# Seven block products for eight in the w_in matmuls of a Fourier layer with two feed-forward layers

## The reference

```python
X = np.fft.rfft(x, axis=1); Xr, Xi = X.real, X.imag
Yr = Xr @ w_r - Xi @ w_i + b_r
Yi = Xr @ w_i + Xi @ w_r + b_i
Y  = soft(Yr, 0.01) + 1j * soft(Yi, 0.01)      # sign(v) * max(|v| - 0.01, 0)
x1 = np.fft.irfft(Y, n=3008, axis=1).reshape(6016, 256)

h = x1 @ w_in                                   # 256 x 2048
x2 = (max(h, 0) + alpha * min(h, 0)) @ w_out    # 2048 x 256
h = x2 @ w_in2
out = where(h >= 1, h, where(h <= -1, 0, (h + 1)**2 / 4)) @ w_out2
```

## Time and profile before

| | |
|---|---|
| median of 3 runs | 1272.91 us (1272.61 to 1273.23) |
| profiled execution | 1272.96 us, of which 1271.4 us span |
| TensorE busy | 98% of the span, mean granted clock 0.992 |
| VectorE, ScalarE, GpSimd busy | 62%, 51%, 5% |

### The profile page before, as it was taken

The page is one execution under the profiler, slowest core; times in us unless marked ns, Lnnn a source line. Parts: engine busy times, 40 slices in busy tenths (PEclk is TensorE's granted clock), DMA queues, the critical chain, the costliest instruction groups (busy, mean ns, idle before and its releaser), DMA issues.

```text
span 1271.4 us, 17546 instructions
## 1 busy us (share of the span) xinstructions
PE 1242.4 (98%) x6304; PEld 1095.8 (86%) x6304; DVE 785.7 (62%) x1389; ACT 649.9 (51%) x1312; POOL 68.4 (5%) x86
## 2 busy tenths in 40 slices
PE   6799999999999999999999999999999999999997
PEld 2689988888888888888888888888888888889997
DVE  2477755666665665666656656666566566666675
ACT  2345455555455455554554554545545545555553
POOL 1355500000000000000000000000000000000000
PEclk9799999999999999999999999999999999999999
DMA  8888810000000000000010000000000000000000
GB/s 262 260 257 258 251 41 16 16 1 1 16 3 29 1 16 16 1 16 16 1 31 1 16 16 1 16 17 1 28 1 13 4 1 16 1 1 16 1 16 28
DMA packets 26684, 54.11 MB, mean 43 GB/s; under 512 B 3018, under 2 KB 15562, under 8 KB 26604
## 3 DMA queue, kind: packets, MB, share of 16 engines
q1 hardware_dynamic: 20660, 31.49, 8.6%
q0 software_dynamic: 4576, 15.67, 3.7%
q10 hardware_dynamic: 1372, 5.97, 1.3%
HBM read 34.37 MB, written 18.74 MB: 42 GB/s over the span
## 4 chain that ended last, share of the span: by engine, by line
PE 96%; DMA 2%; DVE 0%; issue 0%; ACT 0%; SPq 0%; ACTq 0%; POOLq 0%
PE bank L890 82%; PE bank L826 5%; PE bank L873 2%; PE bank L801 2%; PE bank L812 2%; PE bank L836 2%; PE bank L884 1%; DMA x_sb<-x 1%; DMA slots_scratch<-a_sb 1%; DMA gc<-group_consts 1%; SPq L386 0%; ACT act_a L601 0%; PE bank L954 0%; DVE g_sb L753 0%; DVE g_sb L756 0%
## 5 line engine op out<-in xcount | busy, mean ns | idle before, releaser
L890 PE MATMUL bank<-x_hi,w_hi 128*128 128x470 f32 (+1 forms) x832 | 314.8, 378 | 0.9 <-DVE x_lo L716 0.9
L890 PE MATMUL bank<-g_hi,w_lo 128*128 128x470 f32 (+1 forms) x832 | 311.2, 374 | 0.0
L890 PE MATMUL bank<-x_hi,w_lo 128*128 128x470 f32 (+1 forms) x832 | 310.6, 373 | 0.0
L890 PE MATMUL bank<-g_lo,w_hi 128*128 128x470 f32 (+1 forms) x832 | 310.2, 373 | 0.0
L890 PE MATMUL bank<-g_hi,w_hi 128*128 128x470 f32 (+1 forms) x832 | 309.4, 372 | 0.8 <-DVE x_lo L770 0.5
L890 PE MATMUL bank<-x_lo,w_hi 128*128 128x470 f32 (+1 forms) x832 | 308.7, 371 | 0.0
L748 DVE SCALAR_TENSOR_TENSOR g_sb<-act_a,neg_alpha,g_sb 128x470 f32<-128x470 f32 (+1 forms) x208 | 145.8, 701 | 229.6 <-ACT g_sb L599 229.3
L727 DVE TENSOR_TENSOR g_lo<-g_sb,g_hi 128x470 fp32r<-128x470 f32 (+1 forms) x416 | 263.5, 633 | 0.1
L601 ACT ACTIVATE act_a<-bank,half 128x470 f32<-128x470 f32 (+1 forms) x208 | 135.0, 649 | 245.7 <-PE bank L890 245.7
L596 ACT ACTIVATE act_a<-bank 128x470 f32<-128x470 f32 (+1 forms) x208 | 116.2, 559 | 264.8 <-PE bank L890 264.7
L580 ACT ACTIVATE g_hi<-g_sb 128x470 fp32r<-128x470 f32 (+1 forms) x416 | 244.8, 588 | 0.8 <-DVE g_sb L756 0.8
(11 more groups left out here) (50 smaller groups left out, 762.5 us busy)
## 6 DMA issues: line engine op xcount, KB each, us to landing
raw<-wpack POOLq DMA_DIRECT2D x32, 256.0 KB, 4.1
gc<-group_consts SPq DMA_DIRECT2D x24, 256.0 KB, 3.4
slots_scratch<-a_sb POOLq DMA_DIRECT2D x16, 384.0 KB, 6.6
zt<-slots_scratch SPq DMA_DIRECT2D x24, 256.0 KB, 4.4
inverse_scratch<-v_sb SPq DMA_DIRECT2D x24, 256.0 KB, 3.7
out<-rows_out ACTq DMA_DIRECT2D x11, 470.0 KB
x_sb<-x SPq DMA_DIRECT2D x16, 320.0 KB
ut<-inverse_scratch SPq DMA_DIRECT2D x9, 480.0 KB, 4.0
```

What stands on the lines that cost most here:

```text
L890: done = pe.matmul(out_ap, w_of(w), g, start=first and n == 0, stop=last_one and n == 2)
```

## The change

**Layers one behind the other.** All tokens pass layer 1, then all pass layer 2. `x2_all` keeps the result of layer 1 whole in f32. Tiles have N = 376 tokens (4 x 94), 16 of them, taken as 8 pairs per layer.

**Seven products for eight.** A *group* is a pair of tiles (k = 0, 1), one layer and two blocks of 128 hidden values, fp and fp + 8: 8 groups to a pair, 128 groups in all. `w_in`'s part for a group is 2 x 2 blocks (A), the pair's inputs are 2 x 2 blocks (B: two halves of the 256 inputs by two tiles). Before, such four blocks of `h` took eight block products; the change takes seven (P1 to P7, Strassen's scheme in Winograd's form) of 3 matmuls each, of sums A11, A12, A22, S1 to S4 and B11, B21, B22, T1 to T4. The sums of weights are made by GpSimd in the first part (layer 1) and by VectorE (layer 2), those of inputs by VectorE. The four blocks of `h` are C11 (kept in PSUM: P1 and P2 accumulate there) and C22, C21, C12, which VectorE assembles in SBUF: per group one copy and five additions of 376 columns (`make_u2` two, `make_u3`, `make_c22`, `make_c21`, `make_c12`). The w_out products stay as they were: 6 matmuls for each of the four blocks.

**Other engines.** Layer 1's activation is the same three instructions. Layer 2's is relu and square on ScalarE and one max/min on VectorE. `g_hi` stays on ScalarE; `g_lo`, and the low parts of the T sums, go to GpSimd (`low`, `token_lo`). Most operands of the activation are now in SBUF, not PSUM.

**Turning.** TensorE's transposes and VectorE's copies are gone. VectorE transposes 32 x 32 blocks straight from the accumulators into `yt` (`turn`, two instructions per tile, 384 columns each); w_out's columns are reordered on the host to fit. A tile is stored by 12 DMAs on SP's queue, in runs of 64 values (256 bytes); the last tile's by six on SP and six on ACT.

**The first part.** The 48 steps are written out, without hardware loops. `store_a` moves from POOL's queue to ACT's. The weights of layer 1 alone (half of what came in before) are loaded there, on SP's queue, from step 21 on; the first pair's inputs are made in steps 38 to 44; the last mixing and inverses stand inside the first group. The weights of layer 2 are taken in during the last pair of layer 1 and the first of layer 2, in the place of layer 1's: over 16 groups VectorE makes the sums (4 instructions of 128 columns), ScalarE the high and GpSimd the low parts (896 and 512 columns), eight times.

The core of the diff (the new functions run for g = 0 to 128, with out(g - 1) behind the products of g):

```diff
-FTOK = FJ * ROWS            # 5 * 94
+N = JT * ROWS               # 4 * 94
+            def make_p1(g):
...
+                if g:
+                    pe.wait_ge(g_ready, block_no(g - 1, C11) + 1)
+                product(g, c11_bank, A11, B11, last_one=False).then_inc(p1_done, 1)
+            def make_p2(g):
+                pe.wait_ge(p1_left, g + 1)
+                product(g, c11_bank, A12, B21, first=False).then_inc(p2_done, 1)
+            def make_p4(g):
+                pe.wait_ge(u3_ready, g + 1)
+                product(g, c21_bank, A22, T4, first=False).then_inc(p4_done, 1)
+            def make_p3(g):
+                pe.wait_ge(h_ready[C22], g + 1)
+                product(g, c12_bank, S4, B22, first=False).then_inc(p3_done, 1)
+            def make_out(g, nth):
...
+                pe.wait_ge(lo_ready, block_no(g, kind) + 1)
# TensorE, per group
+                    make_p1(g)
+                    make_p6(g)
+                make_out(g - 1, 0)          # C11
...
+                    tokens(q + 1, TOKEN_GROUPS[at])     # layer 1, at = 2 to 5
+                    make_p2(g)
+                    make_p7(g)
+                    make_p5(g)
+                make_out(g - 1, 1)          # C21
+                    make_p4(g)
+                make_out(g - 1, 2)          # C22
+                    make_p3(g)
+                make_out(g - 1, 3)          # C12
# VectorE, per group
+            def make_u2(g):
+                dve.wait_ge(p1_done, g + 1)
...
+                dve.tensor_copy(partial[:, :], c11_bank[:, 0:N]).then_inc(p1_left, 1)
+                dve.wait_ge(p6_done, g + 1)
...
+                dve.tensor_tensor(u2[:, :], partial[:, :], side_bank[:, 0:N], ALU.add).then_inc(u2_ready, 1)
...
+                    make_u2(g)
+                second_part(g - 1, C12)
...
+                    make_u3(g)
+                    make_c22(g)
+                    second_part(g, C11)
...
+                    make_c21(g)
+                    second_part(g, C22)
...
+                    make_c12(g)
+                    second_part(g, C21)
# GpSimd, per group
+                low(g - 1, C22)
+                low(g - 1, C21)
+                lows_first(q + 1, at)
+                take_in_lo(g, 0)
+                low(g - 1, C12)
+                lows_second(q + 1, at)
+                take_in_lo(g, 1)
+                take_out_lo(g)
+                if g < ALL_GROUPS:
+                    low(g, C11)
# ScalarE, per group
+                    first_part(g - 1, C12)
+                high(g - 1, C21)
...
+                    first_part(g, C11)
...
+                high(g - 1, C12)
...
+                    first_part(g, C22)
+                    high(g, C11)
...
+                    first_part(g, C21)
+                    high(g, C22)
# the activation on VectorE: both inputs in SBUF, but for C11 in layer 2
+                    dve.scalar_tensor_tensor(out=gg, in0=a, scalar=neg_alpha[:, f:f + 1], in1=gg,
+                                             op0=ALU.mult, op1=ALU.add).then_inc(g_ready, 1)
...
+                    dve.scalar_tensor_tensor(out=gg, in0=h_of(kind), scalar=1.0, in1=a,
+                                             op0=ALU.max, op1=ALU.min).then_inc(g_ready, 1)
# turning
+                    dve.transpose(yt[k][:, :, :, 32 * c:32 * c + 32], wide).then_inc(acc_left[k][c], 1)
```

More of the change, by code:

```diff
@@ L129, in moved @@
[L129 to L151, removed]
@@ L154, in first_unit @@
[L154 to L168, removed]
@@ L171, in side_use @@
[L171 to L188, removed]
+    return fwd.astype(np.float32), inv.astype(np.float32), pairs.reshape(GROUPS // 2, P, 4 * P).astype(np.float32)
@@ new lines, in x_tile, with a_tile, x2_tile, weight_job @@
+        def x_tile(t):
+            return x_sb[:, t, :]
+        def a_tile(t):
+            return a_sb[:, t, :]
+        def x2_tile(t, c):
+            return x2_all[:, c, t * N:(t + 1) * N]
+        def weight_job(s):
+            n, part = divmod(s - WEIGHT_STEP, 3)
+            return (n, part) if 0 <= n < FP and s >= WEIGHT_STEP else (None, None)
+        def taken(table, g):
+            return table.get(g - TAKE_FROM)
+        def h_of(kind):
+            return c11_bank[:, 0:N] if kind == C11 else h_sb[kind][:, :]
@@ L510, in _ @@
+            for g in range(ALL_GROUPS + 1):
+                q, at = divmod(g, FP)
+                low(g - 1, C22)
[8 more added lines that the diff above has]
+                    low(g, C11)
         @block.scalar
@@ new lines, in high, with keep @@
+            def high(g, kind):
+                if g < 0:
+                    return
+                n = block_no(g, kind)
+                act.wait_ge(g_ready, n + 1)
+                if g:
+                    act.wait_ge(out_done, out_no(g - 1, kind) + 1)
+                act.activation(g_hi[kind][:, :], g_sb[n % 3][:, :], ACT.Copy).then_inc(hi_ready, 1)
+            def keep(q, k):
+                if 0 <= q < TILE_PAIRS:
+                    act.wait_ge(out_done, out_no(FP * q + FP - 1, C21 if k == 0 else C12) + 1)
+                    if q == 0 and k == 0:
+                        for i in range(SLOTS):
+                            act.wait_ge(v_stored[i], 16 * (PAIRS // SLOTS))
+                    act.activation(x2_tile(2 * q + k, 0), acc_bank[k][0][:, 0:N], ACT.Copy)\
+                       .then_inc(acc_left[k][0], 1)
@@ L690, in threshold @@
                 dve.wait_ge(y_clip_ready, s + 1)
-                if not is_early(s, 3):
-                    dve.wait_ge(inv_done, s - 1)
-                dve.tensor_tensor(y_out[slot][:, :], y_sum[:, :], y_clip[:, :], ALU.subtract).then_inc(y_ready, 1)
-            def iteration(i, tiles):
-                for u in range(UNROLL):
-                    s = UNROLL * i + u
-                    split_xt(s, u % SLOTS)
-                    if tiles and has_tile(i, u):
-                        copy_a(tile_at(i, u), a_bank[1])
-                    if not is_early(s, 1):
-                        threshold(s - 1, (u - 1) % SLOTS)
@@ L839, in iteration @@
[L839 to L850 removed]
+                pe.matmul(v_bank[:, 0:D], gc[slot][:, (2 * (s % 2) + 1) * P:(2 * (s % 2) + 2) * P],
+                          y_out[s % SLOTS][:, :], start=True, stop=True).then_inc(inv_done, 1)
@@ new lines, in tokens @@
+            def tokens(q, job):
+                k, c = ((0, 0), (1, 0), (1, 1), (0, 1))[job]
+                pe.wait_ge(u_in[k], 16 * (q + 1))
+                if job:
+                    side_free(q, job)
+                for j in range(JT):
+                    last = pe.matmul(side_bank[:, j * ROWS:(j + 1) * ROWS],
+                                     ut[k][0:ROWS_PAD, j * D + c * P:j * D + (c + 1) * P], inv47[:, :],
+                                     start=True, stop=True)
+                last.then_inc(side_done, 1)
```

1232 lines of the change are left out of this document (729 added, 503 removed).

## The result

The changed kernel takes **1236.13 us** (median of 4 runs, 1235.22 to 1238.44) where the kernel before takes 1273.07 (4 runs, 1272.61 to 1273.23). The ratio is 0.9713, 95% interval 0.9696 to 0.9730: faster by 37 us. 62 were worked out. The profiled execution is the slowest of the four, 1238.44 us with a span of 1236.6.

The account below looks back on a forecast made before the run. The prediction took TensorE's own work to bound the second part and mostly the first. From 1272.96 us, -62.6 - 12.7 - 5 + 2 + 4 + 12 gave 1210.7, so 1211 us, with an 8-in-10 range of 1190 to 1258 us.

Parts of the forecast that it names:

- Matmuls, -62.6: Second part: 5760 matmuls of 376 columns at 171.7 ns take 989.0 us, saving 62.6 us.
- Turning, -12.7: Output turning: TensorE loses its transposes, saving 12.7 us; VectorE's 32 transposes in their place cost nothing.
- Plain groups, +12: Product groups: VectorE and GpSimd excluding each other at the SBUF port costs 12 us, between 0 and 60.
- The walk with exclusion: One group timed with VectorE waiting out each GpSimd low part: one product's slack is used up, but not more.
- Taking in layer 2's weights, +4: Over 16 groups, extra GpSimd and ScalarE work, buffered by 1 to 2 us slack, costs 4 us (0 to 12).
- First part, -5: Before the product groups: no loops, fewer transfers and earlier first inputs save 5 us (-11 to +6).
- `y_out` has about 1.8 us to spare: First-part steps: GpSimd's long instructions can hold y_clip at no cost, upper bound 1 us in each of 8 weight turns.
- End, +2: After the last group: uncovered last blocks and more stores per queue cost 2 us (0 to 6).
- no exclusion for two SBUF inputs: Rival, chance 0.22: VectorE and GpSimd run side by side, TensorE never waits in steady groups; 1199 us.
- GpSimd wins the port each time: Rival, chance 0.17: VectorE slips behind queued low parts, P2 about 1 us late per layer 1 group; 1270 to 1330 us.
- GpSimd fills up in the weight groups: Rival, chance 0.11: ScalarE or GpSimd full in layer 2 and weight groups, half the groups 0.5 us late; say 1240 us.
- The first part gets longer: Rival, chance 0.05: GpSimd's long instructions and SP's weight waits reach TensorE in the first part; 1215 to 1230 us.

Follow-up runs that it names:

- control of experiment 4: Changed kernel with each activation low part on GpSimd replaced by three memsets, about as long as the subtraction but reading nothing: 1214.82 us, ratio 0.9536.
- Experiment 4: Changed kernel with GpSimd filling the activations' low parts with zeros by one memset, which reads nothing, instead of subtracting: 1212.06 us, ratio 0.9518.
- Experiment 5: Changed kernel with y_clip written to PSUM instead of SBUF in 47 of 48 steps of the first part: 1232.06 us, ratio 0.9687.
- the fastest version: Changed kernel with layer 2's weight sums on GpSimd, their low parts on VectorE, and y_clip in PSUM: 1222.13 us, ratio 0.9595.

## Why the prediction was right, and where it was off

The side and the range held (1236.13 in 1190 to 1258), the value was 25 us too low, and just outside the forecast's own range of 1200 to 1230. In part this was luck: the range reached to 1258 for a ScalarE or GpSimd that is full in half of all groups, which didn't come, and what did come, two terms wrong by 25 and 13 us, happened to fit below it. By terms, against the profiled executions (1272.96 and 1238.44):

- **Matmuls, -62.6: right.** Where nothing waits, the matmul is 171.6 ns over 2532 in a row (control of experiment 4), so 5760 cost 988.4 us: **-63.2**. The two runs of 36 were the reading to take. The 172.9 ns of the changed kernel contain waits, which belong to the term of the plain groups.
- **Turning, -12.7.** TensorE's transposes are gone. VectorE's 32 take 556 ns each (the assumption was 0.55 to 1.1) and are hidden, but for their part in the small waits of the next term.
- **Plain groups, +12: +5.** The mechanism is there: the activation's mean rose from 609 ns to 901. The walk with exclusion said that a plain group has room for it, and put the cost on groups in which GpSimd has additional low parts, at half of 1 us each. TensorE waits elsewhere, in the groups in which VectorE has additional work, and loses 0.2 to 0.4 us there.
- **Taking in layer 2's weights, +4: the term that was off most, +29** (27.6 by medians). It was costed as a sum of GpSimd's and ScalarE's work against their room, with the port left to another term. VectorE's four sums weren't given a price at all, as they are short: 4 x 0.28 = 1.1 us. They are 3.5 us by their means (0.94 + 0.94 + 0.97 + 0.69) and 4.5 in the group shown: where one meets a reading GpSimd instruction, it costs about what that one does, whatever its own size. Experiment 4 with its control puts 18 of the 29 us down to the reads of the activations' low parts; the split of the other 11 between the remaining reads and GpSimd's own queue is open.
- **First part, -5: wrong sign, +8.** The first w_in matmul is 5.4 us later than before, the first pair (which has 24 matmuls fewer) takes 3.7 us longer than the others by its matmuls, and the second part has 1.3 us of token instructions fewer, which now stand here. Up to step 21 the changed kernel is ahead by up to 3.9 us, as assumed. The weights' low parts, now long and in pairs, use this up by step 32, and from step 38 on the first inputs come on top. "`y_out` has about 1.8 us to spare" missed that `y_clip` and `y_out` can each wait out a GpSimd instruction in the same step. Experiment 5 takes this away and gains 4.1 us by medians. That the rest is the inputs' additional work on VectorE is argued from the trace: spreading it gained nothing, and no run took it out.
- **End, +2: +1.** The last matmul stands 9.2 us before the end of the span, 9.4 before; the stores are issued more often and hidden in part, and TensorE waits 1.24 us for the last `g_lo`.

1272.96 - 63.2 - 12.7 + 5 + 29 + 8 + 1 is 1240.1; some 2.5 us of stalls in the second part of before are gone: 1237.6, beside 1238.44. The first part's 8 is from one execution of each kernel, and its start varies by some 4 us between the traces here, so the balance is no better than that.

Of the rivals, "no exclusion for two SBUF inputs" is refuted (901 against 629 ns), although in the plain groups the time is within 5 us of what it says. "GpSimd wins the port each time" didn't come: in a plain group neither is starved. "GpSimd fills up in the weight groups" named the place and the size (1240), and it has a part: the wait at 671.97 us is behind GpSimd's own queue, and waits for `g_lo` stay in the control. It isn't the whole, since the control has GpSimd just as full and is 21 us faster. "The first part gets longer" was given 0.05 and holds as well. Exclusion and a longer first part came true at once, which chances for one case each don't provide for.

## What to carry to other kernels

Before moving work to GpSimd, count it together with VectorE's instructions that have two SBUF inputs, as one resource, and count each short one of those at the full length of the GpSimd instruction that it will meet; beside a queue of GpSimd instructions this happens most times (23 of the 32 weight sums here took 0.6 us or more, 9 took 0.28 to 0.29). A way out is to keep one operand or the result of a VectorE instruction in PSUM, which removed the waits here. Giving the short operations to GpSimd and the long ones to VectorE gained 8.9 us; why it did wasn't isolated. Busy shares over a long stretch hide this: look for the few groups with additional work and walk those. TensorE's busy time hides waits of a few tenths of a us too; the distance between starts shows them.

## What the runs showed of the hardware

- A VectorE instruction that meets GpSimd's queue alternates with it: of 128 columns it takes 0.28 us without reading GpSimd instructions beside it, 0.69 to 0.97 us on average with them and 1.08 to 1.25 in the group shown.
- GpSimd memsets of 260 and 376 columns (316 and 414 ns) don't hold VectorE's two-input operations (629 ns).
- `y_clip` with its result in PSUM takes 428 or 429 ns in each of 47 steps where it takes 295 into SBUF alone; so it isn't held by GpSimd.
- In the windows of the exchange, in which TensorE stands idle for about 9 of 60 us, its mean granted clock is 0.97 and 0.98; in the full ones it is 1.00. It falls to 0.50 for some 3 us twice, from 662 and from 778 us, and is 1.00 otherwise. In the run with TensorE 60.00 us busy there it is 1.00 throughout, and so it is in the window of the fastest version, with 6 us idle.
- VectorE transposes 128 x 384 from PSUM in 556 ns, the time of a copy of 376 columns.
